# The sums between the two matmuls of a Strassen-style MLP, made on VectorE instead of on Pool

## The reference

```python
def _attn_ref(q, k, v, g_norm):                     # 8 batches, 8 heads, 576 positions, 64 wide
    kv = np.einsum('bhsd,bhse->bhde', k, v)
    out = np.einsum('bhsd,bhde->bhse', q, kv)
    rms = np.sqrt(np.mean(out * out, axis=-1, keepdims=True) + 1e-06)
    return (out / rms * g_norm).astype(np.float32)

def _moe_ref(x, w_gate, w_val, w_out):              # x 4608x512, d_ff 1536
    gate = 1.0 / (1.0 + np.exp(-(x @ w_gate)))
    val = x @ w_val
    return (gate * val @ w_out).astype(np.float32)

def _moe2_ref(x, w_gate, w_val, w_out):
    g = x @ w_gate
    silu = g * (1.0 / (1.0 + np.exp(-g)))
    val = x @ w_val
    return (silu * val @ w_out).astype(np.float32)

def reference(...):
    # attention output, transposed to x (4608 x 512)
    x = _moe_ref(x=x, **moe_kwargs)
    return _moe2_ref(x=x, **moe2_kwargs)
```

## Time and profile before

| what | value |
|---|---|
| median of 3 runs | 1972.34 us (1971.17 to 1975.84) |
| the profiled execution | 1974.97 us, its span 1973.2 us, mean granted clock 0.99 |
| PE busy | 1844.5 us, 93% of the span |
| DVE busy | 1290.7 us, 65% |
| ACT busy | 877.3 us, 44% |
| POOL busy | 767.8 us, 39% |
| chain that ended last | PE 56%, DVE 18%, issue 9%, POOL 7%, DMA 4%, ACT 4% |

### The profile page before, as it was taken

How to read it: one execution, slowest core, us unless ns; L and a number is a source line. 1 busy time by engine, 2 the same in 40 slices (tenths; PEclk the granted TensorE clock), 3 DMA queues, 4 the chain that set the end, 5 groups by cost and what they waited for, 6 DMA issues and landing times.

```text
span 1973.2 us, 30872 instructions
## 1 busy us (share of the span) xinstructions
PE 1844.5 (93%) x11184; PEld 1769.2 (90%) x11184; DVE 1290.7 (65%) x1773; ACT 877.3 (44%) x1622; POOL 767.8 (39%) x626
## 2 busy tenths in 40 slices
PE   7989899999999999999988899999999998999997
PEld 6878899998999998999988788988899998899997
DVE  2454477776766556766558777777866667766665
ACT  2444355455543334444434444444434434444444
POOL 3454333333533335433346533334422236322222
PEclk9999999999999999999999899999999999999999
DMA  8898254456655566655655344446555555444442
GB/s 210 225 252 250 76 200 182 178 191 214 233 178 176 198 200 208 227 177 185 203 193 179 144 177 176 174 176 226 184 200 198 181 198 198 148 177 177 177 177 80
DMA packets 201464, 370.07 MB, mean 188 GB/s; under 512 B 49761, under 2 KB 160353, under 8 KB 201313
## 3 DMA queue, kind: packets, MB, share of 16 engines
q1 hardware_dynamic: 201312, 368.10, 55.7%
HBM read 235.93 MB, written 132.12 MB: 187 GB/s over the span
## 4 chain that ended last, share of the span: by engine, by line
PE 56%; DVE 18%; issue 9%; POOL 7%; DMA 4%; ACT 4%; SPq 2%; POOLq 0%; DVEq 0%; ACTq 0%
PE ps L579 52%; DVE hop L876 6%; DVE arena L893 3%; DVE arena L906 3%; DVE arena L921 3%; ACT hop L687 2%; DVE xo L827 2%; DMA x<-arena 2%; POOL arena L1064 1%; POOL arena L1094 1%; PE ps L487 1%; DMA wops<-in_moe_w_gate_dram 1%; POOL rrms L1004 1%; PE ps L520 1%; PE ps L467 1%
## 5 line engine op out<-in xcount | busy, mean ns | idle before, releaser
L579 PE MATMUL ps<-xo,wa 128*128 128x384 f32 x6048 | 1090.5, 339 | 49.9 <-DVE arena L893 26.6
L579 PEld LDWEIGHTS ps<-xo,wa 128*128 128x128 f32 x6048 | 1059.0, 190 | 64.1 <-DVE arena L893 37.2
L893 DVE TENSOR_TENSOR arena<-ps,arena 128x384 f32<-128x384 f32 x648 | 351.2, 553 | 399.6 <-PE ps L579 323.5
L579 PE MATMUL ps<-hop,wb 128*128 128x384 f32 x3024 | 559.0, 340 | 42.4 <-DVE hop L876 34.0
L579 PEld LDWEIGHTS ps<-hop,wb 128*128 128x128 f32 x3024 | 523.1, 189 | 74.6 <-DVE hop L876 52.5
L705 ACT ACTIVATE arena<-ps 128x384 f32<-128x384 f32 x648 | 312.9, 490 | 570.7 <-PE ps L579 565.0
L876 DVE TENSOR_TENSOR hop<-arena,hop 128x384 fp32r<-128x384 f32 (+1 forms) x396 | 423.6, 1105 | 73.6 <-ACT hop L687 70.0
L1057 POOL TENSOR_TENSOR arena<-arena 128x384 f32<-128x384 f32 x72 | 73.3, 1018 | 755.0 <-DVE arena L921 754.9
L687 ACT ACTIVATE hop<-arena 128x384 fp32r<-128x384 f32 (+1 forms) x396 | 232.4, 608 | 164.6 <-POOL arena L1057 70.7
L1094 POOL TENSOR_TENSOR arena<-arena 128x384 f32<-128x384 f32 x144 | 145.7, 1036 | 113.3 <-DVE arena L893 113.3
L726 ACT ACTIVATE arena<-arena 128x384 f32<-128x384 f32 x216 | 112.6, 521 | 152.1 <-DVE arena L893 152.1
(11 more groups left out here) (44 smaller groups left out, 988.2 us busy)
## 6 DMA issues: line engine op xcount, KB each, us to landing
xo<-x_operands SPq DMA_DIRECT2D x168, 768.0 KB, 6.2
x_operands<-xo SPq DMA_DIRECT2D x84, 768.0 KB, 3.9
x<-arena SPq DMA_DIRECT2D x120, 384.0 KB, 3.1
arena<-x SPq DMA_DIRECT2D x96, 384.0 KB, 4.4
xraw<-x SPq DMA_DIRECT2D x24, 768.0 KB, 8.3
arena<-in_k_dram SPq DMA_DIRECT2D x32, 288.0 KB, 5.6
arena<-in_v_dram SPq DMA_DIRECT2D x32, 288.0 KB, 6.2
arena<-in_q_dram SPq DMA_DIRECT2D x64, 144.0 KB, 4.0
```

Source lines behind the costliest of these rows:

```text
L579: mm = pe.matmul(dst, lhsT, rhs, start=(pr in (1, 5, 2) and c == 0 and i == 0), stop=(c == 1 and i == 2), skip_group_check=(pr in (6, 7, 4 ...
L893: nc.vector.tensor_tensor(dst, acc, buf, ALU.add).then_inc(summed, 1)
```

## The change

S1, S3, S2 and S4 are issued on VectorE. S1 of a half stands directly behind `hidden(21)` of that half, ahead of `total(12, 1)`. S3 and S2 of a half stand directly behind the `hop_split` of operand (1, c), ahead of that of (5, c): for the first half in window 1, for the second in window 2. S4 stands behind the `hop_split` of (6, 1), ahead of that of (7). The operations, their sizes and the semaphores that they wait for and raise are the same; the wait of S1 for the previous block's splits now stands before both S1.

```diff
+                def hidden_s1(c):
+                    dve.wait_ge(h_done, n_hid(qq, c, 21))
+                    if qq > 0:
+                        dve.wait_ge(hop_lo, len(HOPS) * qq)
+                    nc.vector.tensor_tensor(s14[:, c], h21[:, c], h22[:, c], ALU.add).then_inc(s_made, 1)
+
+                def hidden_s3(c):
+                    dve.wait_ge(s_made, n_s(qq, (S1_0, S1_1)[c]))
+                    nc.vector.tensor_tensor(h21[:, c], h11[:, c], h21[:, c], ALU.subtract).then_inc(s_made, 1)
+
+                def hidden_s2(c):
+                    dve.wait_ge(hop_lo, n_hop(qq, 1, c))
+                    dve.wait_ge(s_made, n_s(qq, (S3_0, S3_1)[c]))
+                    nc.vector.tensor_tensor(h11[:, c], s14[:, c], h11[:, c], ALU.subtract).then_inc(s_made, 1)
+
+                def hidden_s4():
+                    dve.wait_ge(hop_lo, n_hop(qq, 5, 1))
+                    dve.wait_ge(h_done, n_hid(qq, 1, 12))
+                    dve.wait_ge(s_made, n_s(qq, S2_1))
+                    nc.vector.tensor_tensor(s14, h12, h11, ALU.subtract).then_inc(s_made, 1)
...
                             hop_split(1, 0)
+                            hidden_s3(0)
+                            hidden_s2(0)
                             hop_split(5, 0)
...
                         hidden(21)
+                        hidden_s1(w)
                         total(12, 1)
...
                         hop_split(1, 1)
+                        hidden_s3(1)
+                        hidden_s2(1)
                         hop_split(5, 1)
                         hop_split(2, 1)
                         hop_split(6, 1)
+                        hidden_s4()
                         hop_split(7, None)
...
                 if first_unit is not None:
                     differences(first_unit)
                     differences(first_unit + 1)
                 if blk == 0 and qq > 0:
                     differences(6 * (qq // NB) + 4)
                     differences(6 * (qq // NB) + 5)
-                hidden_s1(0)
                 if prepares:
                     x_s1_s3(nxt)
-                hidden_s3_s2(0)
                 if prepares:
                     x_s2(nxt)
                     x_s4(nxt)
-                hidden_s1(1)
-                hidden_s3_s2(1)
-                pool.wait_ge(hop_lo, n_hop(qq, 5, 1))
-                pool.wait_ge(h_done, n_hid(qq, 1, 12))
-                pool.wait_ge(s_made, n_s(qq, S2_1))
-                nc.gpsimd.tensor_tensor(s14, h12, h11, ALU.subtract).then_inc(s_made, 1)
                 if first_unit is not None:
                     differences(first_unit + 2)
                     differences(first_unit + 3)
```

More of the change, by code:

```diff
@@ L1050, in _ @@
                 first_unit = 6 * (qq // NB + 1) if blk == NB - 1 and nxt < QN else None
-                def hidden_s1(c):
-                    pool.wait_ge(h_done, n_hid(qq, c, 21))
-                    if c == 0 and qq > 0:
-                        pool.wait_ge(hop_lo, len(HOPS) * qq)
-                    nc.gpsimd.tensor_tensor(s14[:, c], h21[:, c], h22[:, c], ALU.add).then_inc(s_made, 1)
-                def hidden_s3_s2(c):
-                    pool.wait_ge(s_made, n_s(qq, (S1_0, S1_1)[c]))
-                    nc.gpsimd.tensor_tensor(h21[:, c], h11[:, c], h21[:, c], ALU.subtract).then_inc(s_made, 1)
-                    pool.wait_ge(hop_lo, n_hop(qq, 1, c))
-                    pool.wait_ge(s_made, n_s(qq, (S3_0, S3_1)[c]))
-                    nc.gpsimd.tensor_tensor(h11[:, c], s14[:, c], h11[:, c], ALU.subtract).then_inc(s_made, 1)
                 if first_unit is not None:
```

## The result

The changed kernel takes 1912.95 us (median of 4 runs, 1909.56 to 1915.1), the kernel before 1971.76 on the same chip: a ratio of 0.9696, 95% [0.9676, 0.9716], or 58.8 us less. Forecast were 1893 in a range of 1866 to 1926. So the sign, the place and the range held, and a quarter of the forecast gain is missing (79 us forecast). The profiled execution took 1909.56, the lowest of the four, its span 1907.8, against a span of 1973.2 before.

What follows compares the result with a forecast made beforehand. PE, busy 93%, was taken as the bound, losing time to DVE splits held by Pool's sums. Gains by block kind summed to 79.5 us off the profiled 1974.97, giving 1895.5, forecast as 1893 us; eight in ten 1866 to 1926.

Steps and rivals of the forecast that it cites:

- rival 3: DVE becomes the bound between splits (1, 1) and (6, 1), above 0.78 us an operation: slower, 2027 us; chance 0.04.
- signs of being wrong: S3 and S2 averaging above 0.78, blocks with weight units not shortening, or PE waiting for `total(12)`, which S1 now precedes.
- rivals, 2: Blocks 17 and 18 keep their clock, late blocks' totals leave PE's way wholly: 107 us gain, 1865 us; chance 0.11.
- Rival 4: All blocks: the wait only moves, PE waiting as long for (5, 1) as for (6, 1); within 5 us; chance 0.04.
- Rival 1: Pool's differences and x sums take the cover; 19 blocks with such work gain only 1.1 each: 1927 us; chance 0.15.
- plain, layer 0 (8): Window 2: (5, 1) and (6, 1) ready in time, 1.1 us in each of 8 blocks, 9 us.
- plain layer 1 and turning (9): Window 2: gain 1.6 us each, with a new 0.3 wait for the split of (5, 1); 14.5 us.
- prepares x, layer 0 (5): Totals and `hidden(21)` earlier by 1.2 us, then 1.57 more over 27 PE steps: 2.8 each, 14 us.
- prepares x, layer 1 (4): Blocks 19 to 22: `total(22, 1)` moves by 0.65, then 1.6 in window 2: 2.2 each, 9 us.
- last of a pass (4): Blocks 5, 11, 23, 29: S1 leaves Pool's queue, early differences cost 2: net 2.7 each, 11 us.
- first of a pass (4): Blocks 6, 12, 24, 30: 0.8 in window 1, 1.5 to 2.1 in window 2: 2.6 each, 10.5 us.
- 17 and 18: ACT's long wait for S1 shortens: 5.6 + 1 in block 17, 3.5 + 1.5 in block 18; 11.5 us.

Runs made afterwards that it cites:

- spare_read: The changed kernel plus five unused Pool sums per block that read SBUF, at the old places of the second half's S1, S3, S2 and S4: 1951.5 us.
- late_diff: The changed kernel, but Pool's second pair of weight differences waits for S4: 1903.28 us.
- split51_first: The changed kernel, but in window 2 the split of (5, 1) stands ahead of S3 and S2: 1911.19 us.
- changed_again: The changed kernel run again unaltered, as the reference on another chip: 1913.44 us.
- best: The changed kernel with second differences behind S4, window 2's split of (5, 1) before S3 and S2, ACT's product 1 copies before (6, 1)'s high part: 1901.04 us.

## Why the prediction was right, and which terms were mis-sized

The mechanism held as it was put: the splits fell to 0.63 (0.65 to 0.8 forecast), PE's waits for them from 34.0 to 6.4 us (below 8), S3 and S2 have means of 0.66 and 0.73 (the threshold of rival 3 was 0.78), DVE is busy 67%. Of the 21 waits that are left, 16 sit before step 8 in layer 1, as forecast, but they are only 3.3 of the 6.4 us; the other five, 3.1 us, are in blocks 5, 11 and 29, beside the differences. ACT's wait for a sum in block 17 is gone, but a wait of 3.81 for a difference stands in its place. One of the signs of being wrong did show, in small: PE waits for `total(12, 1)` in blocks 23 and 29, 0.15 and 0.27 us, where it did not before. The row is the tenth matmul of window 2 of block 29, which is product 5:

```profile
1589.76 1.86 PE L579 MATMUL ps<-hop,wb 128*128 128x384 f32 x9 [0.27 <-DVE arena L915]
```

S1 stands ahead of that total and takes 1.09 there, beside a difference. It is the risk that the prediction named, at a cost of tenths.

`spare_read` shows by itself that holding, and not the length of Pool's own sums, is enough for the loss in window 2. Of the rivals, 2 and 3 did not come. Rival 4 is there as a remainder of 0.5 us a block in layer 1, not as a wait of the old size. Rival 1 is the one that took a part: the blocks with other work gave less than forecast, though they gave more than the 1.1 it left them.

Term by term, from the starts of the two profiled executions (us):

| blocks | forecast | measured |
|---|---|---|
| plain, layer 0 (8) | 9 | 8.9 |
| plain layer 1 and turning (9) | 14.5 | 12.6 |
| prepares x, layer 0 (5) | 14 | 13.4 |
| prepares x, layer 1 (4) | 9 | 7.3 |
| last of a pass (4) | 11 | 6.2 |
| first of a pass (4) | 10.5 | 6.3 |
| 17 and 18 | 11.5 | 7.6 |
| sum | 79.5 | 62.3 |

The other 3.1 us of the span's 65.4 are the attention stage, which ends at 219.6 in the one and 216.55 in the other and lay between 216.55 and 222.65 in the profiles of all kernels; it is not the change's. The profiled before was 3.2 above its median and the profiled after 3.4 below its own, hence 58.8 between the medians.

- *The three terms with weight work, 12.9 of the 17.2 us that are missing.* For the last blocks of a pass I took ranges and summed at their upper end, for the first blocks in the middle, and for 17 and 18 I took single values. In the last blocks of a pass windows 0 and 1 gave 2.37, 2.50, 0.98 and 2.01 (2 to 2.7 forecast), and window 2 had 1.5 at most to give in layer 0 (16.04 to 14.56) where I wrote 1.5 to 2. Without the second differences it gives 1.3 to 1.4 each, and they take back 7.05 in all by `late_diff`. So the charge for them was right in total (8 forecast), wrong in place: 2.5 in blocks 5 and 11, 0.5 in 23, 1.6 in 29. Adding up: 7.9 + 5.3 − 7.05 = 6.2.
- *First blocks.* Window 2 gave 1.3 to 1.4, not 1.5 to 2.1: 1.5 was all that it could give in layer 0, and 1.0 stayed in layer 1. Windows 0 and 1 gave 0.7 in blocks 6 and 12 as forecast (0.8), but −0.5 and 0.1 in 24 and 30. Window 1 of block 24 is as long as before, 16.34 us: `total(11, 0)` stands behind `split_w` on DVE, which waits 1.29 us for ACT, and this ACT work stands behind a copy that PE's pace sets. No sum was on that path. The 0.5 is lost in window 0, ahead of it, where PE's wait for `silu` grew from 0.82 to 1.27: the weight DMA lets Pool's second differences start 0.76 us after the end of the first ones (1.31 before), and they now hold two operations of DVE's chain (1.10 and 0.97 us) where they held one (0.54 and 1.08). That is holding again, set by when a DMA lands; windows 0 and 1 of block 24 gave 1.0 in the profile of `split51_first`.
- *17 and 18.* Windows 0 and 1 of block 17 gave 3.4, not 5.6: ACT's long wait became one of 3.81 for the differences, but behind it PE waits twice more, and the clock falls behind the first wait as it did before (0.66 and 0.63). The first wait fell by 4.3, but the second, 2.06 for an ACT copy, is new, and the working had none there. Block 18 gave 2.0, not 3.5.
- *Plain layer 1.* The eight blocks with a loss of 1.9 were to give 1.6, with 0.3 left at step 8. 0.5 stays there, and they gave 1.4; block 25, with its 2.1, gave 1.6. This 0.2 in nine blocks is the whole 1.9 us of the term, and the other layer-1 blocks lack it too.
- *x in layer 1.* Windows 0 and 1 gave 2.6, the forecast; window 2 gave 4.8 of 6.4, in `changed_again` 3.4. Of the 1.6 that are missing, 0.9 is what stays at step 8 (blocks 19 and 20 gave 1.4 each); the rest is the clock in blocks 21 and 22, of which the last section tells.

## What to carry to other kernels

A Pool operation that nobody waits for long can still set the pace: look in the timeline for DVE operations that are longer than their free price and end a fixed time after a Pool operation (0.41 to 0.43 us here), and move the holder, not the held. Moving it to DVE costs a free operation each and gives back the held part of all the others, so a DVE busy at 65% can get less busy by taking more, as it did here (1290.7 to 1269.9 us). When work leaves a queue, look at what stood behind it there: it now starts early, and may have to be held back by a wait on purpose; and cap each block's gain by what the block has to lose against PE's pace before adding it up.

## What the runs showed of the hardware

The price of a chain step on DVE depends on what is waited for. Independent operations of 384 columns start 0.47 us apart. One that needs the one before it starts 0.58 after it in some pairs and 0.66 in others, with hardly any spread in the changed kernel's trace: 0.57 to 0.59 from `silu` to `hidden` in layer 1 and from `hidden(21)` to S1, 0.65 to 0.66 from `total` to `hidden` in layer 0 and from S3 to S2 (1411.14 to 1411.80, and 278.40 to 279.05). All four kinds wait on two semaphores. In the cheap pairs the one that the instruction before raises is waited for first, in the dear ones second. Whether exchanging the two waits of S2 would save the 0.07 was not tried.

Window 2 of blocks 19 to 22 takes 15.2 or 16.1 to 16.4 us in one and the same kernel. Windows of `best` on PE alone (PE busy, then PEclk, DMA share, GB/s), block 19 and then block 20:

```profile
1121.30:1125.00 3.70, 3.57 (x19) 1.00 0.30 120
1168.20:1170.00 1.80, 1.80 (x6) 0.57 0.57 229
1170.00:1172.00 2.00, 2.00 (x9) 0.53 0.00 0
```

In both blocks PE had just waited twice, 0.97 and 1.05 us in block 19, 0.98 and 1.07 in block 20, the second wait 2.4 us after the first. Then it ran at 2.4 GHz in block 19 and near the 1.2 GHz level for some 3.5 us in block 20, which cost 1.1. Which of these four blocks are hit changes from run to run, and what decides it stays open.
